# Tap sums of chunk 0 on TensorE for six tokens instead of four, with the last channels of two tokens on its two column halves, and chunk 1's first tap sum begun by VectorE between chunk 0's rounds

## The reference

```
w = exp(weight_gen - max over k);  w = w / (sum over k + 1e-9)
attn[b, s, h, g] = sum over k of w[b, s, h, k] * x_pad[b, s + k, h, g]      # k = 0..6, six rows of zeros ahead
h = relu(attn @ w_in)                                                       # 192 -> 1024
conv[s] = conv_w[0] * h[s-1] + conv_w[1] * h[s] + conv_w[2] * h[s+1]
out = (h * sigmoid(conv)) @ w_out                                           # 1024 -> 192
```

## Time and profile before

| | us |
|---|---|
| median of 3 runs (718.36 to 718.83) | 718.39 |
| profiled execution, its own time | 718.5 |
| its span | 716.7 |
| TensorE busy | 706.4 (99%) |
| VectorE busy | 614.3 (86%) |
| GpSimd busy | 614.2 (86%) |
| ScalarE busy | 497.3 (69%) |

### The profile page before, as it was taken

One profiled execution on the slowest core, in us unless ns is written; L12 is line 12 of the kernel. 1 busy time (PEld: TensorE's weight loads), 2 busy tenths in 40 slices (PEclk: granted clock), 3 DMA queues, 4 the chain that ended last, 5 costly groups with the idle time before them and its releaser, 6 DMA issues.

```text
span 716.7 us, 9863 instructions
## 1 busy us (share of the span) xinstructions
PE 706.4 (99%) x3839; PEld 634.6 (89%) x3839; DVE 614.3 (86%) x549; ACT 497.3 (69%) x636; POOL 614.2 (86%) x285
## 2 busy tenths in 40 slices
PE   8997999999999999999999999999999999999998
PEld 8756889899999999999989898989899999999997
DVE  7998999999988989898898989898999989885630
ACT  3658867696767676776977676677777867676641
POOL 5999999999997999999899999989898899925310
PEclk9999999999999999999999999999999999999999
DMA  8420312103031222212030210203020200000001
GB/s 239 145 104 1 91 51 77 44 22 100 18 100 30 72 60 55 86 36 95 23 101 16 69 50 23 93 23 108 27 93 23 50 21 20 23 18 23 23 29 34
DMA packets 26297, 41.44 MB, mean 58 GB/s; under 512 B 3864, under 2 KB 23678, under 8 KB 24461
## 3 DMA queue, kind: packets, MB, share of 16 engines
q1 hardware_dynamic: 26250, 40.81, 18.7%
HBM read 28.02 MB, written 12.78 MB: 57 GB/s over the span
## 4 chain that ended last, share of the span: by engine, by line
PE 95%; ACT 2%; DVE 2%; issue 0%; DMA 0%; SPq 0%; ACTq 0%
PE out_ps L952 45%; PE z L930 41%; PE turn_ps L974 3%; PE turn_ps L952 2%; PE z L942 1%; PE z L991 1%; PE turn_ps L991 0%; PE out_ps L991 0%; ACT hidden L634 0%; PE z L952 0%; DVE z L773 0%; DVE z L779 0%; ACT gated L653 0%; DMA logits<-in_weight_gen 0%; DVE xb L824 0%
## 5 line engine op out<-in xcount | busy, mean ns | idle before, releaser
L486 POOL TENSOR_TENSOR weighted<-x_win,soft 128x1344 f32<-128x1344 f32 (+1 forms) x128 | 351.1, 2764 | 7.4 <-DMA x_win<-in_x 7.3
L952 PE MATMUL out_ps<-wo,gated 128*128 128x192 f32 x2000 | 346.0, 326 | 0.2
L952 PEld LDWEIGHTS out_ps<-wo,gated 128*128 128x128 f32 x2000 | 326.9, 190 | 8.4 <-ACT out_sb L689 0.8
L603 POOL TENSOR_TENSOR gated<-gated,hidden 128x1022 f32<-128x1022 f32 (+1 forms) x117 | 248.4, 2123 | 73.9 <-ACT gated L653 73.7
L773 DVE SCALAR_TENSOR_TENSOR z<-hidden,cw,z 128x1022 f32<-128x1022 f32 (+1 forms) x134 | 164.6, 1229 | 59.8 <-ACT z L640 59.0
L634 ACT ACTIVATE hidden<-z 128x1024 f32<-128x1024 f32 (+1 forms) x136 | 134.5, 989 | 106.5 <-PE z L930 99.0
L779 DVE SCALAR_TENSOR_TENSOR z<-hidden,cw,z 128x1022 f32<-128x1022 f32 (+1 forms) x134 | 166.2, 1240 | 4.2
L640 ACT ACTIVATE z<-hidden,cw 128x1022 f32<-128x1022 f32 (+1 forms) x134 | 144.9, 1081 | 4.2
L814 DVE TENSOR_REDUCE attn_a<-weighted 128x256 f32<-128x1792 f32 (+1 forms) x62 | 124.8, 2012 | 0.0
L653 ACT ACTIVATE gated<-z 128x1022 f32<-128x1022 f32 (+1 forms) x117 | 115.1, 984 | 12.0 <-PE out_ps L952 7.1
L930 PE MATMUL z<-xa_hi,wa_hi 128*128 128x512 f32 (+1 forms) x264 | 100.1, 458 | 5.4 <-ACT gated L653 5.2
(11 more groups left out here) (83 smaller groups left out, 394.6 us busy)
## 6 DMA issues: line engine op xcount, KB each, us to landing
x_win<-in_x SPq DMA_DIRECT2D x11, 1344.0 KB, 6.4
out<-out_sb SPq DMA_DIRECT2D x111, 96.0 KB
logits<-in_weight_gen SPq DMA_DIRECT2D x12, 224.0 KB
x_win<-in_x SPq DMA_DIRECT2D x2, 1008.0 KB
out<-out_sb SPq DMA_DIRECT2D x16, 84.0 KB
x_win<-in_x SPq DMA_DIRECT2D x1, 1176.0 KB
x_win<-in_x SPq DMA_DIRECT2D x1, 768.0 KB, 10.1
wo<-in_moe_w_out SPq DMA_DIRECT2D x1, 768.0 KB, 13.9
```

The source lines that it names most:

```text
L486: return engine.tensor_tensor(to, rows, s, ALU.mult)
L603: nc.gpsimd.tensor_tensor(gated_flat(c, n), gated_flat(c, n), hidden[:, n % 3, 1:1 + c.size], ALU.mult) \
L952: last = nc.tensor.matmul(bank[0:end - begin, 0:D], gated[:, j, begin:end], wo[:, j, :], start=(j == 0), stop=(j == J - 1))
```

## The change

`BY_TENSOR` grows by tokens 4 and 6, and `SUMS_FIRST` shrinks to 0 and 2. GpSimd's products of 4 and 6 are laid out tap by tap, as those of VectorE are. The rounds of the last channels become kind "b": the first half of a round's tokens on partitions 0 to 63, the second half on 64 to 127. `sum_and_turn_last(i)` sums the last 64 channels of tokens i and i + 2 with alternating matmuls on these two column halves; tokens 0 and 2 are turned by one matmul each in the same form. The remainders of the weights now come behind all four rounds, on TensorE and on ScalarE. VectorE shifts chunk 2's logits before the low parts and does `sum_taps` of chunk 1, index 0, after the second. GpSimd's product 4 of chunk 1 waits until TensorE has read the products 4 and 6, whose places it takes.

```diff
-ROUNDS_FIRST = [[("a", 0, 4)], [("single", 0, 4)], [("a", 4, 8)], [("single", 4, 8)]]
+ROUNDS_FIRST = [[("a", 0, 4)], [("b", 0, 4)], [("a", 4, 8)], [("b", 4, 8)]]
-BY_TENSOR = (1, 3, 5, 7)
-SUMS_FIRST = (0, 2, 4, 6)
+BY_TENSOR = (1, 3, 4, 5, 6, 7)
+SUMS_FIRST = (0, 2)
...
+                if c is CHUNKS[1] and i == FIRST.half:
+                    pool.wait_ge(s_turned, rounds_before(c))
                 multiply(nc.gpsimd, c, i, soft).then_inc(s_weighted, 1)
...
             take_turned(FIRST, 1)
-            take_rest(0, wa_lo)
             take_turned(FIRST, 2)
             take_turned(FIRST, 3)
+            take_rest(0, wa_lo)
             take_rest(1, wb_lo)
...
                 for c, i in SUM_AT.get(k, []):
-                    sum_taps(c, i)
+                    if c is not CHUNKS[1] or i:
+                        sum_taps(c, i)
...
                 for i in SUMS_FIRST:
                     sum_taps(c, i)
+                shift(CHUNKS[2])
                 low_part(c, 0)
-                shift(CHUNKS[2])
                 low_part(c, 1)
+                sum_taps(CHUNKS[1], 0)
                 low_part(c, 2)
                 low_part(c, 3)
...
-                    if n == 0 and m in (2, 4):
-                        pe.wait_ge(s_weights_lo, m - 1)
+                    if n == 0 and m in (0, 4):
+                        pe.wait_ge(s_weights_lo, max(m - 1, 1))
...
+                        if c is FIRST and kind == "b" and i not in BY_TENSOR:
+                            for u, rows in ((i, slice(0, D2)), (i + half, slice(D2, P))):
+                                last = nc.tensor.matmul(bank_of(c, r)[rows, at * c.parts:(at + 1) * c.parts], attn_first[:, u, P:D],
+                                                        ident[0:c.parts, 0:c.parts], start=True, stop=True)
...
+            def sum_and_turn_last(i):
+
+                c, at = FIRST, i % 4
+                product_ready(i)
+                product_ready(i + 2)
+                bank = bank_of(c, i // 4 * 2 + 1)
+                if bank is soft_bank:
+                    pe.wait_ge(s_weighted_dve, len(BY_VECTOR))
+                for tap in range(K):
+                    for u, rows in ((i, slice(0, D2)), (i + 2, slice(D2, P))):
+                        taps = places(c, u, 1)[:, 0].rearrange("p (k d) -> p k d", k=K)
+                        last = nc.tensor.matmul(bank[rows, at * c.parts:(at + 1) * c.parts], taps[:, tap, P:D],
+                                                ident[0:c.parts, 0:c.parts], start=(tap == 0), stop=(tap == K - 1))
+                return last
...
             sum_and_turn(1)
             sum_and_turn(3)
+            sum_and_turn_last(1)
             turn_conv_weights()
-            for i in BY_TENSOR[2:]:
-                sum_and_turn(i)
+            sum_and_turn(5)
+            sum_and_turn(4)
+            sum_and_turn(7)
+            sum_and_turn_last(5)
             turn(FIRST, 0)
             turn(FIRST, 1)
+            sum_and_turn(6).then_inc(s_turned, 1)
+            sum_and_turn_last(4).then_inc(s_turned, 1)
             rest_of_weights(0, wa_hi, stage_a)
-            turn(FIRST, 2)
-            turn(FIRST, 3)
```

More of the change, by code:

```diff
@@ L260, in summed_before @@
     def summed_before(place):
-        first = [SUMS_FIRST.index(i) + 1 for i in range(FIRST.tokens) if i not in BY_VECTOR][:place]
+        first = [SUMS_FIRST.index(i) + 1 for i in range(FIRST.tokens) if i in SUMS_FIRST][:place]
         here = place - place_of(CHUNKS[1], 0)
@@ L276, in operations @@
                 at += stop - first
[L277 to L283 removed]
+            else:
+                half = (stop - first) // 2
+                found.append((slice(0, D2), slice(first, first + half), at, half))
+                found.append((slice(D2, P), slice(first + half, stop), at, half))
+                at += half
         return found
@@ L293, in summed_for @@
         if c is FIRST:
-            return max(SUMS_FIRST.index(i) + 1 for kind, first, stop in c.rounds[r] for i in range(first, stop) if i not in BY_TENSOR)
+            return max(SUMS_FIRST.index(i) + 1 for kind, first, stop in c.rounds[r] for i in range(first, stop) if i in SUMS_FIRST)
         return sums_before(c, max(stop - (kind == "a") for kind, first, stop in c.rounds[r]))
@@ L967, in turn @@
                 for kind, first, stop in c.rounds[r]:
-                    for i in range(first, stop) if kind != "b" else range(first // 2, stop // 2):
+                    half = (stop - first) // 2
+                    for i in range(first, stop) if kind == "a" else range(first, first + half):
                         if c is not FIRST:
@@ L977, in turn, with product_ready @@
                 last.then_inc(s_turned, 1)
-            def sum_and_turn(i):
-                c = FIRST
-                pe.wait_ge(s_weighted_dve, BY_VECTOR.index(i) + 1)
-                for r, pieces in enumerate(c.rounds):
-                    for kind, first, stop in pieces:
-                        if first <= i < stop:
-                            channels = slice(0, P) if kind == "a" else slice(D - P, D)
-                            taps = places(c, i, 1)[:, 0].rearrange("p (k d) -> p k d", k=K)[:, :, channels]
-                            if bank_of(c, r) is soft_bank:
-                                pe.wait_ge(s_weighted_dve, len(BY_VECTOR))
-                            for tap in range(K):
-                                nc.tensor.matmul(bank_of(c, r)[:, (i - first) * c.parts:(i - first + 1) * c.parts], taps[:, tap, :],
-                                                 ident[0:c.parts, 0:c.parts], start=(tap == 0), stop=(tap == K - 1))
+            def product_ready(i):
+                if i in BY_VECTOR:
+                    pe.wait_ge(s_weighted_dve, BY_VECTOR.index(i) + 1)
+                else:
+                    pe.wait_ge(s_weighted, products_before(FIRST, i + 1))
@@ new lines, in sum_and_turn @@
+            def sum_and_turn(i):
+                c, at = FIRST, i % 4
+                product_ready(i)
+                taps = places(c, i, 1)[:, 0].rearrange("p (k d) -> p k d", k=K)
+                for tap in range(K):
+                    last = nc.tensor.matmul(bank_of(c, i // 4 * 2)[:, at * c.parts:(at + 1) * c.parts], taps[:, tap, 0:P],
+                                            ident[0:c.parts, 0:c.parts], start=(tap == 0), stop=(tap == K - 1))
+                return last
+            def sum_and_turn_last(i):
+                c, at = FIRST, i % 4
+                product_ready(i)
+                product_ready(i + 2)
+                bank = bank_of(c, i // 4 * 2 + 1)
+                if bank is soft_bank:
+                    pe.wait_ge(s_weighted_dve, len(BY_VECTOR))
+                for tap in range(K):
+                    for u, rows in ((i, slice(0, D2)), (i + 2, slice(D2, P))):
+                        taps = places(c, u, 1)[:, 0].rearrange("p (k d) -> p k d", k=K)
+                        last = nc.tensor.matmul(bank[rows, at * c.parts:(at + 1) * c.parts], taps[:, tap, P:D],
+                                                ident[0:c.parts, 0:c.parts], start=(tap == 0), stop=(tap == K - 1))
+                return last
```

4 lines of the change are left out of this document (2 added, 2 removed).

## The result

| | before | after |
|---|---|---|
| median, us | 718.38 (718.25 to 719.10, 6 runs) | 721.53 (720.61 to 723.06, 6 runs) |
| ratio after / before | | 1.0041, 95% interval 1.0031 to 1.0051 |
| profiled execution, us | 718.5 | 721.26 (span 719.5) |

The changed kernel is slower by 3.15 us between the medians and by 2.8 us between the two profiled executions. The forecast was 5.1 us later; the sign and the range held, the size did not.

What follows compares the result with a forecast made beforehand. TensorE's work before 31 us was taken to set the end. Remainder start 22.15 + 88c = 29.50, plus 6.93, put step 0's fifth part at 36.43 against 31.30: 5.1 us later, 723.5 us; range 719.9 to 726.2.

Steps and rivals of the forecast that it cites:

- first rival: Narrow rows at the start: both halves fully at once, c = 0.056, 2.7 us later, 721.1 us; 22 in 100.
- What bounds the start: TensorE's unbroken work before 31 us: every microsecond added there goes through to the end; VectorE's sums count as nothing.
- fourth rival: VectorE, not TensorE, sets the stretch to 55 us; two sums removed gain up to 2.94 us, 715.5 us; 9 in 100.
- c, the price of a narrow row: TensorE's time per 64-column row on alternating halves: 0.0835 us taken, between bounds 0.056 and 0.112, for 88 rows.
- The load in proportion to its columns: TensorE's weight loads: 0.84 ns a column, so 64 columns save 54 ns of the 0.11 us a load holds up.
- Switching: TensorE going to narrow matmuls and back costs 0.30 us, done four times at the start: 1.20 us.
- The exposed wait: TensorE idles 0.68 us before token 3, whose product is ready at 12.71, with nothing between tokens 1 and 3.
- The sum: TensorE's remainder of the weights starts at 22.15 + 88c = 29.50; step 0's fifth part 6.93 us later, at 36.43.
- Costs set at nothing: GpSimd's new wait for product 4 of chunk 1, four half-width ScalarE evictions, VectorE's moved sum (up to 2.0 us uncovered).
- Given back later: TensorE's 0.3 us free between 30 and 58 us may return up to that much; left out of the forecast.
- third rival: Full overlap, free switches, some of the 0.3 us given back: 1.3 us later, 719.7 us; 15 in 100.
- the second: Rival with no overlap of the halves, c = 0.112: 7.6 us later, 726.0 us; 18 in 100.

Runs made afterwards that it cites:

- half_by_half: Changed kernel, but each block does all seven taps of one token on its half, then all seven of the other; 724.36 us, ratio 1.0082.
- tokens_0_2: Changed kernel, but TensorE sums tokens 0 and 2 instead of 4 and 6, which VectorE sums; 720.46 us, ratio 1.0028.
- sum_back_0_2: tokens_0_2 with chunk 1's first sum back in its old place behind the low parts; 720.47 us against 720.46.
- moved_sum_before: Kernel before, with only VectorE's first sum of chunk 1 moved between the second and third low part; 719.94 us, ratio 1.0033.
- the repeat: The changed kernel timed once more without any edit; 721.31 us, ratio 1.0042.
- the filling: Matmuls that nobody reads, put into TensorE's waits; in the changed kernel 3 between tokens 1 and 3: 721.08 us, ratio 1.0037.
- four_early: tokens_0_2, but TensorE sums only tokens 0 to 3; chunk 1's sum, the remainder's first part and its rounding where before has them; 722.41 us, ratio 1.0047.
- four_halves: Changed kernel, but TensorE sums only tokens 1, 3, 5, 7, VectorE four; chunk 1's first sum not moved; 718.82 us, profiled 717.42.
- exposed_before: Kernel before, but TensorE does the first 128 channels of tokens 1 and 3, then the last channels of both; 718.91 us, ratio 1.0008.

## Why the prediction was right in sign and off in size

- **Luck in the range.** The median of 721.53 us lies below the 722.2 to 723.8 that the forecast gave its own mechanism (32 in 100), and within 0.5 us of the first rival's 721.1 (22 in 100). The range held because it spanned the rivals.
- **What bounds the start.** Right in the main. TensorE's added work before 31 us reaches the end: 2.81 us at step 0's fifth part, 2.72 at the entry to the steady stretch. Where the work is less (halves alone), the end comes earlier. The fourth rival (VectorE sets the stretch) falls: its 2.8 us less of work turned into 3.70 us of waiting. But one sentence was wrong: "Nobody that sets the end waits for VectorE there". In before, step 0 waits for VectorE's last low part (29.32), and ScalarE's rounding, which the forecast put on the path, had ended at 31.17, 0.13 us before the fifth part. In after it is the rounding. The 3.00 us served for both, since the two ways are nearly of one length, which the forecast had not seen. Nor do eight transposes stand ahead of 23.93 but four; the sum does not use them.
- **The step that failed: c, the price of a narrow row.** Taken 0.0835, measured 0.0545 us. 88 rows by 0.029 are 2.6 us, which is more than the whole difference of the forecast (2.3 us at the fifth part, 36.43 against 34.11). What happened is the first rival: both halves at once. The lower bound, 0.056, was a little high. The reasoning took one rule of the wide rows, that the load of the next weights starts only with the matmul before it, and held it across the halves. It holds within a half (loads 0.109 us apart in half_by_half); the load for the other half starts 6 ns after. The upper bound, 0.112, is nearly what half_by_half shows, 2.82 us for 28 rows or 0.10 a row. The Trainium skill (TensorEngine Tiling (Array Packing), Key Properties) says that different tiles can load weights and multiply in parallel. The trace agrees (loads 6 ns apart, matmuls 7 ns apart). The forecast had set that rule beside its sum, with the first rival.
- **The load in proportion to its columns** held: 64 columns take 137 ns in after, where the line through the earlier trace rows gives 136. But since the load hides behind the other half's matmul, it sets nothing.
- **Switching.** Predicted four times 0.30. From token 3's start to the remainder are 14.35 us; five wide groups at 1.5625, the convolution weights 0.16, two transposes 0.22 and 88 rows by 0.0545 are 12.99. The 1.36 left are four times 0.34 (put down to switching as what is left over, not measured alone). They are spread: 0.46 in the three blocks (1.68 against 28 x 0.0545 = 1.53), 0.30 in the turns of tokens 0 and 2 (22.97 to 23.71, 0.74 against 0.44), the rest in wide groups beside narrow work, 1.65 to 1.76 us from start to start instead of 1.56 (token 3's is 1.76, 12.80 to 14.56).
- **The exposed wait.** Predicted 0.68 us, seen 12.80 less 12.09, 0.71. tokens_0_2 gives 0.69 back.
- **The sum.** 22.15 + 88 x 0.0545 = 26.95, measured 27.15. From there 4.03 + 2.93 us against 3.93 + 3.00. So with c right the sum would have given 33.88 for the fifth part, seen 34.11. Step 0 began at 31.90, not near 34, and the steady stretch at 76.50, not near 78.9; blocks took 1.68 us, the first rival's 1.6.
- **Costs set at nothing** were nothing: GpSimd's wait, the evictions of half width (ScalarE stands idle 1.56 us behind the last of them, until TensorE's remainder), the moved sum (sum_back_0_2). That the last rests on cover, moved_sum_before shows.
- **Given back later:** 0.17 us, at chunk 0's fourth step (2.88 us later than before at the end of its first three steps, 2.71 from then on). The forecast allowed up to 0.3.
- **The third rival** (free switches) falls with the 1.36 us; the second (no overlap) needs the other order of the loops.
- Between the medians it is 3.15 us, 0.4 more than between the profiles. In the repeat it is 2.85 and with the filling 2.71, so this part comes from the spread of after's runs and may be chance.

## What to carry to other kernels

Before two column halves are priced, ask in which order they are issued: alternating, a pair costs one row's time, and one half after the other costs nearly as much as full width. Work is worth moving only off the engine without idle time in that stretch; here the halves brought the end forward by about 1 us in the profiled execution, and the two tokens put on TensorE in exchange took 3.8. When an engine's new pause is on the path, look at the granted clock of several runs: a pause may cost more than its length, and a few matmuls that nobody reads held it in the two kernels where it fell most often.

## What the runs showed of the hardware that was not expected

- In kernels with a new pause of 1.4 to 2.4 us between 23 and 31 us, TensorE's clock fell in some runs: in 9 of 12 of four_early (pause of 2.1 to 2.4 us), 6 of 12 of four_halves (1.36), 2 of 5 of moved_sum_before (1.60). It fell too in 2 of 11 of after and its repeat, whose pause before token 3 is 0.7 to 0.8 us, and in none of exposed_before's 11, where that pause is 1.05 us (these from start to start). It cost 1.3 to 4.6 us, mostly more than the pause itself. With unread matmuls in the pauses all 27 runs stayed at 1.0; for after, 5 runs against 2 falls in 11 prove nothing. Where one fall was profiled it is the 1.2 GHz level; of the other runs only the mean clock is known, so that the fall came behind the named pause is argued there, and shown by the filling for four_early and four_halves alone.
- The length of a pause does not decide it alone. TensorE's timeline of before:

```profile
62.96 0.69 PE L930 MATMUL z<-xa_hi,wa_hi 128*128 128x512 f32 x2 [1.73 <-ACT gated L653]
```

  This pause and one of 1.59 us four us later stand in before, ahead of the unread matmuls that it already has at 69.5 us, and its 65 runs in the three sessions all had a clock of 1.0. What makes the pauses between 23 and 31 us different no run shows.
- The Trainium skill (TensorE: Matmul & The Clock Gate, What's actually happening) has 1.2 GHz as the level of an idle engine and activity as what lifts it; the level agrees with the 0.50 from 26.7 to 33.5 us above.
- The load of x lands at different times in different executions: the product that waits for it started between 10.59 and 11.61 us in twelve profiles. An order that leaves it uncovered hands that on to the end (11.61 in exposed_before, lag 1.1; the same 11.60 in tokens_0_2, where token 0's rows cover it, and token 3 starts without a pause).
- VectorE took 2.58 us for a product of 128x1344 written with the taps innermost, and 1.50 written straight. Whether all of that is the layout was not measured by itself.
- Open stays how much of after's spread of 2 us went with the 3 unread matmuls, which hide a load up to 0.14 us later than the profiled one, and how much with the session: all profiles of session three have a load of x that came early (11.01 us at the latest), and there were only 5 runs.
